# Second MoE: destinations looked up ahead of the gather, and no weight chunk split for an expert that does not exist

## The chip, the cores and the metric

The kernel runs on one core of one Trainium2 chip. The metric is the device time of one execution in microseconds; the time before is 440.69 us, the median of three runs (439.51 to 441.41).

## What is computed

Attention with a local window and global keys (4 x 768 tokens, 8 heads of 64), a soft MoE over its output, and then a second, hard-routed MoE, in which the change lies. All in fp32:

```
def _moe2_ref(x, w_gate, w1, w2):            # x 3072 x 512, 8 experts, F = 1024
    logits = x @ w_gate
    expert_idx = np.argmax(logits, axis=1)
    ...
    gate_w = probs[np.arange(N), expert_idx]
    for e in range(E):
        mask = expert_idx == e
        if not mask.any():
            continue
        xe = x[mask]
        h = np.maximum(xe @ w1[e], 0.0)
        out[mask] = gate_w[mask, None] * (h @ w2[e])
```

## The kernel before

All sizes of the second MoE are found on the chip. Experts that have tokens are numbered by **rank** 0 to used-1. A rank's tokens are cut into **units** of 256 tokens, two **tiles** of 128 each; a rank's last unit may hold only one tile. On these inputs the trace shows 26 scalings (13 units) and 25 stores, and two splits at a rank's end: there are two ranks, the first of 12 units (u = 0 to 11) and the second of one unit (u = 12) with one tile. Every engine runs its own loop over ranks (outer) and units (inner, `u = first + j`), and they meet only in semaphores.

**TensorE** (PE), per unit u: `tile(u, 0)` (8 groups `fc` of 3 matmuls on lines 1626 to 1628, into `Yq[0]`; after `fc == 1` it turns the gathered rows of unit u+1, `turn(u + 1)`, line 1546, which waits for `gathered`), then `hidden(u + 1)` (8 matmuls, line 1557), then `tile(u, 1)`. In `tile(u, 0)` each even `fc` waits for `hid_low` of its quarter of the hidden layer; the last of these waits is before `fc == 6`.

**ScalarE** (ACT): copies the turned rows out (`turned_out`), fetches the folded weights of a coming unit, and makes the four quarters `hh` of the next unit (`relu`, line 1724). At the end of a rank it splits chunks of 128x1024 weights, `raw` to `w2h` (line 1788).

**VectorE** (DVE), per unit: `scaled(u, 0)`, `low(u+1, 0..2)` (line 1913, the low part of the hidden layer, which TensorE waits for as `hid_low`), `scaled(u, 1)`, `low(u+1, 3)`. `scaled` waits until the store before has landed (`stored`), adds one to `row_free`, waits for TensorE's tile, and writes `Ysb` (line 1986). There is one `Ysb`, so a tile's scaling always comes behind the landing of the tile before it. At the end of a rank VectorE forms `w2l` of the chunks that ScalarE split (line 2011).

**GpSimd** (POOL), per unit: `gather(u + 2)`: copy two columns of source rows (`src1`, line 1480), wait for the copy and for `turn(u + 1)`, and issue two indirect DMAs of 128 rows (line 1486). Then for each tile: wait for `row_free`, copy one column of destinations (`dst1`, line 1509), wait for the copy and for `y_scaled`, and issue the indirect store of `Ysb` (line 1513).

How many chunks are split at a rank's end is `chunks_at_end`: four if there is an expert of rank + 2, and otherwise one. ScalarE's one chunk waits for the last quarter of the rank's last tile, VectorE's one for ScalarE's.

Of the kernel before, what the change touches and what calls it, by code (L numbers as in the profile page):

```python
# [15 lines left out]
F32 = mybir.dt.float32  # L16
F32R = mybir.dt.float32r
I32 = mybir.dt.int32
BF16 = mybir.dt.bfloat16
ALU = mybir.AluOpType  # L20
# [3 lines left out]
P = 128  # L24
# [12 lines left out]
TOK = BATCH * SEQ  # L37
# [22 lines left out]
W2CH = 4  # L60
# [1163 lines left out]
def top1_moe(nc, ctx, sb, psum, sem, block, sp_passed, ident, ones, Rsel, wg_sb, mem, STR, CT, counting,  # L1224
# [7 lines left out]
    st = ExitStack()  # L1232
# [4 lines left out]
    dst_i = sb(st, "dst_i", [P, MAXT], I32)  # L1237
# [7 lines left out]
    Ysb = spare[:, 0:D]  # L1245
    Gpart = spare[:, WSIZE - 4 * 512:].rearrange("p (n f) -> p n f", f=512)
    Gall = mem[:, 2:4, :].rearrange("p a (b f) -> p (a b) f", f=F)
    w2h = sb(st, "w2h", [P, 2, WSIZE], F32R)
    w2l = sb(st, "w2l", [P, 2, WSIZE], F32R)
# [2 lines left out]
    Cg = sb(st, "Cg", [P, 2, P])  # L1252
    CgT = sb(st, "CgT", [P, 2 * P], F32R)
    src1 = sb(st, "src1", [P, 2], I32)
    dst1 = sb(st, "dst1", [P, 1], I32)

    GWs = sb(st, "GWs", [P, REP, NE])
    own_rows = sb(st, "own_rows", [P, REP])
# [10 lines left out]
    act = sb(st, "act", [P, NE])  # L1269
# [34 lines left out]
    raw = mem[:, 0, :]  # L1304
# [38 lines left out]
    v2_loaded = [sem("v2_loaded_first"), sem("v2_loaded_second")]  # L1343
# [3 lines left out]
    w2_high = sem("w2_high")  # L1347
    w2_low = sem("w2_low")
    src_copied = sem("src_copied")
    dst_copied = sem("dst_copied")  # L1350
# [6 lines left out]
    y_quarter = sem("y_quarter")  # L1357
    y_first = sem("y_first")
    y_scaled = sem("y_scaled")
    stored = sem("stored")  # L1360
    row_free = sem("row_free")
    g_here = sem("g_here")
    g_kept = sem("g_kept")
    act_passed = sem("act_passed")
    dve_passed = sem("dve_passed")
    pool_step = sem("pool_step")
    tokens_hot = sem("tokens_hot")

    def column(t):

        return t if isinstance(t, int) else t.with_bounds(min_val=0, max_val=MAXT - 2)
# [5 lines left out]
    def rank_at(r):  # L1377

        return r if isinstance(r, int) else r.with_bounds(min_val=0, max_val=NE - 1)
# [5 lines left out]
    def plan(eng, r):  # L1385

        word = eng.value_load(rt[0:1, 1, bass.ds(rank_at(r), 1)], min_val=0, max_val=(1 << 19) - 1)
        return ((word & 15).with_bounds(min_val=1, max_val=TT // 2),
                ((word >> 4) & 31).with_bounds(min_val=0, max_val=MAXU - 3),
                ((word >> 9) & 31).with_bounds(min_val=1, max_val=TT),  # L1390
                (word >> 14).with_bounds(min_val=0, max_val=TT + NE - 2))

    def count(eng):

        return eng.value_load(rt[0:1, 2, 0:1], min_val=1, max_val=NE)

    def all_units(eng):

        return eng.value_load(rt[0:1, 2, 1:2], min_val=1, max_val=MAXU - 2)

    def all_tiles(eng):

        return eng.value_load(rt[0:1, 2, 2:3], min_val=1, max_val=TT + NE - 1)

    def chunks_at_end(rank, used):


        return 1 + (rank + 2 < used) * (W2CH - 1)

    def chunk(ch):  # L1410

        return slice(ch * CW, (ch + 1) * CW) if isinstance(ch, int) else bass.ds(ch * CW, CW)
# [50 lines left out]
    @block.gpsimd  # L1463
    def _(pool):
        pool.sem_inc(y_quarter, 4)
        pool.sem_inc(y_scaled, 2)
        pool.wait_ge(c_stored, 16)
        pool.wait_ge(first_ready, 1)

        def gather(u, turned):  # L1470


            if not isinstance(u, int) or u >= 1:
                pool.wait_ge(gathered, u * 32)
                pool.sem_inc(pool_step, 1)
            if isinstance(u, int):
                index = src_i[:, 2 * u:2 * u + 2] if u else src_0[:]
            else:
                index = src1[:]
                nc.gpsimd.tensor_copy(src1[:], src_i[:, bass.ds(column(u * 2), 2)]).then_inc(src_copied, 1)  # L1480
                pool.wait_ge(src_copied, u - 1)
            if not isinstance(u, int) or u >= 1:
                pool.wait_ge(cg_turned, turned)
            pool.sem_inc(pool_step, 1)
            for i in range(2):
                nc.gpsimd.indirect_dma_start(out=Cg[:, i, :], out_offset=None, in_=c_dram,  # L1486
                                             in_offset=bass.IndirectOffsetOnAxis(ap=index[:, i:i + 1], axis=0)
                                             ).then_inc(gathered, 16)

        gather(0, 0)  # L1490
        pool.wait_ge(v2_half, 16)
        nc.gpsimd.tensor_copy(w2h[:, 0, chunk(0)], w2l[:, 0, chunk(0)].bitcast(F32)).then_inc(w2_first, 1)
        pool.wait_ge(src_ready, 1)
        gather(1, 1)
        pool.wait_ge(rt_ready, 1)
        pool.wait_ge(dst_ready, 1)
        used, total = count(pool), all_tiles(pool)
        with pool.Fori(0, used) as rank:
            units, first, tiles, tile0 = plan(pool, rank)
            with pool.Fori(0, units) as j:  # L1500
                u = first + j
                gather(u + 2, u + 2)

                with pool.Fori(0, 1 + (tiles > j * 2 + 1)) as i:
                    done = tile0 + j * 2 + i

                    pool.wait_ge(row_free, u * 2 + i + 1)
                    pool.sem_inc(pool_step, 1)
                    nc.gpsimd.tensor_copy(dst1[:], dst_i[:, bass.ds(column(u * 2 + i), 1)]).then_inc(dst_copied, 1)
                    pool.wait_ge(dst_copied, done + 1)  # L1510
                    pool.wait_ge(y_scaled, u * 2 + i + 3)
                    pool.sem_inc(pool_step, 1)
                    nc.gpsimd.indirect_dma_start(  # L1513
                        out=out_d, out_offset=bass.IndirectOffsetOnAxis(ap=dst1[:, 0:1], axis=0),
                        in_=Ysb, in_offset=None, bounds_check=TOK - 1, oob_is_err=False
                    ).then_inc(stored, 16)

        pool.wait_ge(stored, total * 16)
        pool.sem_inc(pool_step, 1)
        units = all_units(pool)  # L1520
        pool.wait_ge(gathered, (units + 2) * 32)
        pool.sem_inc(pool_step, 1)
# [166 lines left out]
    def _(act):  # L1689
# [3 lines left out]
        used = count(act)  # L1693
# [86 lines left out]

        def rank_done(rank, last):

            act.wait_ge(v2_loaded[1], (rank + 1) * (rank + 2 < used) * 16 + 16)
            act.sem_inc(act_passed, 1)
            act.wait_ge(y_quarter, last * 4 + 4)
            act.sem_inc(act_passed, 1)
            with act.Fori(0, chunks_at_end(rank, used)) as ch:
                nc.scalar.copy(w2h[:, bass.ds(rank & 1, 1), chunk(ch)].rearrange("p a f -> p (a f)"),
                               raw[:, chunk(ch)]).then_inc(w2_high, 1)

        act.wait_ge(v1_loaded[1], 16)
        for ch in range(W2CH):
# [1 line left out]
        with act.Fori(0, used) as rank:  # L1794
            units, first = plan(act, rank)[0:2]

            with act.If(units > (rank < 1) * 1):
                with act.Fori((rank < 1) * 1, units) as j:
                    u = first + j
# [4 lines left out]
    def _(dve):  # L1804
        v = nc.vector
# [140 lines left out]
        step(v.tensor_reduce(tr_f[:], past[:], AX, ALU.add))  # L1946
        v.tensor_scalar(tr[:], tr_f[:], float(NE - 1), None, ALU.min).then_inc(rt_ready, 1)

        used = count(dve)

        dve.wait_ge(r_exp, 1)
# [21 lines left out]
        def scaled(u, i, done):  # L1973

            if isinstance(done, int):
                if done:
                    dve.wait_ge(stored, done * 16)
            else:
                with dve.If(done > 0):
                    dve.wait_ge(stored, done * 16)  # L1980
                    dve.sem_inc(dve_passed, 1)
            dve.sem_inc(row_free, 1)
            dve.wait_ge(*((y_quarter, u * 4 + 8) if i else (y_first, u + 1)))
            dve.sem_inc(dve_passed, 1)
            at = u * 2 + i
            v.tensor_scalar(Ysb, Yq[i][:], gate_s[:, at:at + 1] if isinstance(u, int) else  # L1986
                            gate_s[:, bass.ds(column(at), 1)], None, ALU.mult).then_inc(y_scaled, 1)
# [7 lines left out]
        with dve.Fori(0, used) as rank:  # L1995
            units, first, _, tile0 = plan(dve, rank)

            with dve.If(units > (rank < 1) * 1):
                with dve.Fori((rank < 1) * 1, units) as j:
                    u = first + j  # L2000
                    scaled(u, 0, tile0 + j * 2)
                    for q in range(3):
                        low(u + 1, q)
                    scaled(u, 1, tile0 + j * 2 + 1)
                    low(u + 1, 3)
            with dve.Fori(0, chunks_at_end(rank, used)) as ch:

                all_done = (rank + 1 < used) + (used < 2)
                dve.wait_ge(w2_high, rank * W2CH + W2CH + 2 + ch + all_done * (W2CH - 1))
                dve.sem_inc(dve_passed, 1)  # L2010
                v.tensor_tensor(w2l[:, bass.ds(rank & 1, 1), chunk(ch)].rearrange("p a f -> p (a f)"), raw[:, chunk(ch)],
                                w2h[:, bass.ds(rank & 1, 1), chunk(ch)].rearrange("p a f -> p (a f)").bitcast(F32),
                                ALU.subtract).then_inc(w2_low, 1)

    st.close()

# [43 lines left out]
```

## Time and profile before

| | us |
|---|---|
| median of three runs | 440.69 |
| lowest, highest | 439.51, 441.41 |
| the profiled execution, its device time | 439.07 |
| its span on the core | 437.40 |
| second MoE's loop over units, from the first store | 287.07 to the end |
| PE busy in the span | 421.4 |
| DVE, ACT, POOL busy | 239.2, 212.2, 210.0 |

The rows below give times in us from the span's start. A timeline row is start, duration, engine, line, operation, output<-input, and in brackets how long the engine had been idle and what released it. A DMA row of POOL is the time in which GpSimd works on the issue, not the transfer. DVEq and POOLq are the sequencers of these engines, which handle semaphores and registers.

### The profile page before, as it was taken

The numbers are of one execution on the slowest core, as the hardware profiler recorded it, in microseconds if no ns is written. First come the engines' busy times: TensorE is split into PE (matmuls) and PEld (weight loads), VectorE is DVE, ScalarE is ACT, GpSimd is POOL, SyncE is SP. The second block draws the span as 40 slices with busy tenths as digits, with TensorE's granted clock in tenths as the row PEclk, the third lists the DMA queues.
The fourth block names the chain that finished last, engine by engine and source line by source line (L and its number), as shares of the span: only waits on it lengthen the run. The fifth ranks groups of instructions, "written<-read, shape, count | busy, mean of one in ns | idle before, by whom it ended". The sixth has DMA issues, their size and how long they took to land.

```text
span 437.4 us, 9412 instructions
## 1 busy us (share of the span) xinstructions
PE 421.4 (96%) x3036; PEld 353.6 (81%) x3037; DVE 239.2 (55%) x791; ACT 212.2 (49%) x418; POOL 210.0 (48%) x216
## 2 busy tenths in 40 slices
PE   8999999999999999998797999999999999999996
PEld 7899999999999997743234977688888888888884
DVE  6667777777767775556100679574333323333344
ACT  3887788788888773422010016373333333332244
POOL 5899999999999910010001020234333344443422
PEclk9999999999999999999999999999999999999999
DMA  7866989898977304999995488511111111112111
GB/s 236 278 220 251 402 345 393 343 364 317 393 262 240 106 21 133 391 391 409 397 386 211 140 294 289 217 55 60 60 53 43 60 60 60 60 36 58 55 54 14
DMA packets 29174, 89.21 MB, mean 204 GB/s; under 512 B 3440, under 2 KB 6000, under 8 KB 29136
## 3 DMA queue, kind: packets, MB, share of 16 engines
q1 hardware_dynamic: 25456, 78.47, 48.4%
q0 software_dynamic: 3360, 9.83, 7.2%
q10 hardware_dynamic: 320, 0.42, 0.4%
q8 instruction: 22, 0.36, 0.3%
q14 instruction: 16, 0.13, 0.1%
HBM read 80.85 MB, written 8.13 MB: 203 GB/s over the span
## 4 chain that ended last, share of the span: by engine, by line
PE 85%; DMA 7%; DVE 3%; issue 2%; ACT 1%; POOL 0%; SPq 0%; ACTq 0%; DVEq 0%; POOLq 0%
PE O L445 17%; PE Yq L1626 11%; PE Yq L1627 10%; PE Yq L1628 10%; PE PT L427 9%; PE S L418 5%; PE S L417 5%; DMA ext<-in_moe_w 5%; PE Gp L1557 3%; DMA w2h<-in_moe_w 2%; PE XTp L893 2%; PE Lp L982 2%; PE Cp L1529 2%; PE O L395 2%; PE Up L902 1%
## 5 line engine op out<-in xcount | busy, mean ns | idle before, releaser
L523 ACT ACTIVATE shared<-shared,nm 128x256 f32<-128x256 f32 (+1 forms) x192 | 83.7, 484 | 30.3 <-DVE nm L636 30.1
L445 PE MATMUL O<-V,PTs 128*128 128x65 f32 x704 | 90.1, 269 | 0.0
L636 DVE CUSTOM_DVE_ANT_0 shared<-S,TA 128x256 f32<-128x256 f32 (+1 forms) x192 | 68.7, 396 | 34.4 <-PE S L418 31.7
L445 PEld LDWEIGHTS O<-V,PTs 128*128 128x128 f32 x704 | 86.5, 191 | 1.1 <-issue 1.0
L1626 PE MATMUL Yq<-w2h,hh 128*128 x208 | 83.0, 399 | 0.4 <-issue 0.4
L1627 PE MATMUL Yq<-w2l,hh 128*128 x208 | 81.2, 390 | 0.0
L1628 PE MATMUL Yq<-w2h,hl 128*128 x208 | 81.2, 390 | 0.0
L380 POOL TENSOR_TENSOR kl<-k_raw,kh 128x816 fp32r<-128x816 f32 x30 | 57.9, 1931 | 5.0 <-ACT kh L538 2.9
L1913 DVE SCALAR_TENSOR_TENSOR hl<-Gp,hh 128x512 fp32r<-128x512 f32 x56 | 38.1, 688 | 39.4 <-ACT hh L1724 39.4
L376 POOL TENSOR_TENSOR qs<-q_raw,qs 64x768 fp32r<-64x768 f32 x30 | 54.7, 1825 | 2.4
L427 PE MATMUL PT<-ident,shared 128*128 128x128 f32 x352 | 54.7, 274 | 0.0
L417 PE MATMUL S<-kh,qs 128*128 128x256 f32 (+1 forms) x180 | 53.0, 317 | 0.0
L1724 ACT ACTIVATE hh<-Gp 128x512 fp32r<-128x512 f32 x56 | 32.9, 600 | 30.4 <-PE Yq L1628 27.4
L1986 DVE TENSOR_SCALAR mem<-Yq,gate_s 128x512 f32<-128x512 f32 x26 | 19.5, 751 | 49.7 <-PE Yq L1628 47.0
L1626 PEld LDWEIGHTS Yq<-w2h,hh 128*128 128x128 f32 x208 | 39.1, 188 | 9.2 <-issue 1.5
L418 PE MATMUL S<-kl,qs 128*128 128x256 f32 (+1 forms) x180 | 46.2, 280 | 0.0
L1628 PEld LDWEIGHTS Yq<-w2h,hl 128*128 128x128 f32 x208 | 39.0, 188 | 8.3
L1627 PEld LDWEIGHTS Yq<-w2l,hh 128*128 128x128 f32 x208 | 39.2, 188 | 7.4 <-issue 0.2
L1486 POOL DMA_INDIRECT Cg<-c_rows,src x28 | 27.6, 986 | 35.2 <-DVE src L1892 19.6
L1513 POOL DMA_INDIRECT out<-mem,dst x25 | 25.5, 1019 | 37.4 <-DVE mem L1986 34.4
L1736 ACT CAST Gst<-mem 128x512 fp32r x28 | 16.0, 617 | 54.7 <-PE Gp L1557 53.3
L427 PEld LDWEIGHTS PT<-ident,shared 128*128 128x128 f32 x352 | 42.1, 156 | 0.3 <-ACT shared L523 0.3
(248 smaller groups left out, 571.7 us busy)
## 6 DMA issues: line engine op xcount, KB each, us to landing
mem<-in_moe_w SPq DMA_DIRECT2D x9, 2048.0 KB, 11.6
ext<-in_moe_w SPq DMA_DIRECT2D x6, 2048.0 KB, 19.8
V<-in_v SPq DMA_DIRECT2D x16, 715.0 KB, 6.8
k_raw<-in_k SPq DMA_DIRECT2D x13, 816.0 KB, 7.0
q_raw<-in_q SPq DMA_DIRECT2D x13, 768.0 KB, 4.6
xmem<-in_moe_w SPq DMA_DIRECT2D x2, 2048.0 KB, 11.1
w2h<-in_moe_w SPq DMA_DIRECT2D x1, 2048.0 KB, 10.2
w2l<-in_moe_w SPq DMA_DIRECT2D x1, 2048.0 KB, 15.5
```

The costliest lines, as they stand in the source:

```text
L376: nc.gpsimd.tensor_tensor(qs[HD:P, buf, :, cq], q_raw[HD:P, buf, :, cq], qs[HD:P, buf, :, cq].bitcast(F32), ALU.subtract).then_inc(q_split, 1)
L380: nc.gpsimd.tensor_tensor(kl[:, buf, :, ck], k_raw[:, buf, :, ck], kh[:, buf, :, ck].bitcast(F32), ALU.subtract).then_inc(k_split, 1)
L417: pe.matmul(S[par][h][:, 0:w], q, kh[:, buf, h, at:at + w], start=True, stop=False)
L418: mm = pe.matmul(S[par][h][:, 0:w], q, kl[:, buf, h, at:at + w], start=False, stop=True)
L427: mm = pe.transpose(PT[par][:, (h * kbs + kb) * P:(h * kbs + kb + 1) * P], Pb[:, par, h, kb * P:(kb + 1) * P], ident[:])
L445: mm = pe.matmul(O[grp % 2][:, at:at + VC], PTs[:, par, (h * kbs + kb) * P:(h * kbs + kb + 1) * P], V[:, buf, h, vb, :], start=(n == 0), s ...
L523: nc.scalar.activation(Pb[:, par, h, 0:width(g)], Pb[:, par, h, 0:width(g)], ACT.Exp, bias=nm[:, par, h:h + 1], scale=-1.0).then_inc(exp_d ...
L636: v.tensor_tensor_reduce(Pb[:, par, h, 0:w], S[par][h][:, 0:w], tab, -SCALE, HUGE, ALU.add, ALU.min, nm[:, par, h:h + 1]).then_inc(biased, 1)
L1626: pe.matmul(Yq[i][:], h, high[:, cols], start=(fc == 0), stop=False)
L1627: pe.matmul(Yq[i][:], h, low[:, cols], start=False, stop=False)
L1628: mm = pe.matmul(Yq[i][:], rest, high[:, cols], start=False, stop=(fc == FC - 1))
L1913: v.scalar_tensor_tensor(hl[:, q, :], Gp[:, q, :], 0.0, hh[:, q, :].bitcast(F32), ALU.max, ALU.subtract).then_inc(hid_low, 1)
```

## The change

GpSimd's loop over a unit's tiles is written out. At the start of a unit it waits for `row_free` of the unit's first tile (the landing of the last store of the unit before), copies two columns of destinations at once, then runs `gather(u + 2)`, then the stores; the second store has no copy and no wait for `row_free` any more. So that the first unit doesn't wait for its own tile, VectorE adds the first `row_free` ahead of the loop. `chunks_at_end` goes away: ScalarE and VectorE split four chunks if there is an expert of rank + 2, and otherwise none.

```diff
-    dst1 = sb(st, "dst1", [P, 1], I32)
+    dst1 = sb(st, "dst1", [P, 2], I32)
...
+        def store(i):
+            nc.gpsimd.indirect_dma_start(
+                out=out_d, out_offset=bass.IndirectOffsetOnAxis(ap=dst1[:, i:i + 1], axis=0),
+                in_=Ysb, in_offset=None, bounds_check=TOK - 1, oob_is_err=False).then_inc(stored, 16)
...
             with pool.Fori(0, units) as j:
                 u = first + j
+                pool.wait_ge(row_free, u * 2 + 1)
+                pool.sem_inc(pool_step, 1)
+                nc.gpsimd.tensor_copy(dst1[:], dst_i[:, bass.ds(column(u * 2), 2)]).then_inc(dst_copied, 1)
                 gather(u + 2, u + 2)
-                with pool.Fori(0, 1 + (tiles > j * 2 + 1)) as i:
-                    done = tile0 + j * 2 + i
-                    pool.wait_ge(row_free, u * 2 + i + 1)
...
-                    pool.wait_ge(dst_copied, done + 1)
-                    pool.wait_ge(y_scaled, u * 2 + i + 3)
...
+                pool.wait_ge(dst_copied, u + 1)
+                pool.wait_ge(y_scaled, u * 2 + 3)
+                pool.sem_inc(pool_step, 1)
+                store(0)
+                with pool.If(tiles > j * 2 + 1):
+                    pool.wait_ge(y_scaled, u * 2 + 4)
                     pool.sem_inc(pool_step, 1)
+                    store(1)
...
         def rank_done(rank, last):
-            act.wait_ge(v2_loaded[1], (rank + 1) * (rank + 2 < used) * 16 + 16)
...
-            with act.Fori(0, chunks_at_end(rank, used)) as ch:
+            with act.If(rank + 2 < used):
...
+                for ch in range(W2CH):
...
+        dve.sem_inc(row_free, 1)
         used = count(dve)
...
-            dve.sem_inc(row_free, 1)
+            if not isinstance(done, int) or done:
+                dve.sem_inc(row_free, 1)
...
-            with dve.Fori(0, chunks_at_end(rank, used)) as ch:
+            with dve.If(rank + 2 < used):
+                for ch in range(W2CH):
```

GpSimd, the body of the loop over units, before. `src` and `dst` are `src1` and `dst1`, the first two DMAs the gather, `out<-mem` the store:

```order
L1480 COPY src<-src_i 128x2
L1481 REGISTER_ALU
L1486 DMA Cg<-c_rows,src 128x128 [waits src_copied,cg_turned]
L1486 DMA Cg<-c_rows,src 128x128
L1504 UNCONDITIONAL_BRANCH
L1504 ISA
L1509 ISA [waits row_free]
L1509 COPY dst<-dst_i 128x1
L1510 ISA
L1511 REGISTER_ALU [waits dst_copied]
L1513 DMA out<-mem,dst 3072x512 [waits y_scaled]
```

The same place after:

```order
L1506 ISA [waits row_free]
L1506 COPY dst<-dst_i 128x2
L1469 ISA
L1475 ISA [waits gathered]
L1475 COPY src<-src_i 128x2
L1476 REGISTER_ALU
L1481 DMA Cg<-c_rows,src 128x128 [waits src_copied,cg_turned]
L1481 DMA Cg<-c_rows,src 128x128
L1509 REGISTER_ALU [waits dst_copied]
L1487 DMA out<-mem,dst 3072x512 [waits y_scaled]
```

The wait for `row_free` and the copy of destinations moved from behind the two gather DMAs to ahead of them, and nothing but a register operation is left between the gather and the first store.

ScalarE, the end of the loop over ranks, before (`w2h<-mem` is the split of a chunk of `raw`):

```order
L1785 REGISTER_ALU [waits v2_loaded_second]
L1785 REGISTER_ALU
L1785 ISA
L1787 UNCONDITIONAL_BRANCH [waits y_quarter]
L1787 ISA
L1788 REGISTER_ALU
L1788 ISA
L1788 COPY w2h<-mem 128x1024
```

The same place after:

```order
L1784 REGISTER_ALU
L1784 COMPARE_AND_BRANCH
L1785 ISA
L1787 REGISTER_ALU [waits v2_loaded_second]
L1787 REGISTER_ALU
L1787 ISA
L1790 REGISTER_ALU [waits y_quarter]
L1790 ISA
L1790 COPY w2h<-mem 128x1024
```

A branch now stands ahead of the waits and the copy, and jumps over all of it for the last two ranks; VectorE's end of a rank is changed in the same way.

## Rows read from the trace of the kernel before

**Rows 1.** The page: PE's share of the span, and the chain that ended last.
```profile
PE 421.4 (96%) x3036; PEld 353.6 (81%) x3037; DVE 239.2 (55%) x791; ACT 212.2 (49%) x418; POOL 210.0 (48%) x216
...
PE 85%; DMA 7%; DVE 3%; issue 2%; ACT 1%; POOL 0%; SPq 0%; ACTq 0%; DVEq 0%; POOLq 0%
```

**Rows 2.** The chain that ended last, its final pieces: start, us, what.
```profile
432.87 0.24 PE Yq L1628
...
434.31 1.05 ACT w2h L1788
...
435.87 1.22 DVE w2l L2011
```

**Rows 3.** Timeline, VectorE at the end: last scaling, last `low`, the chunk's low half.
```profile
433.35 0.75 DVE L1986 TENSOR_SCALAR mem<-Yq,gate_s 128x512 f32<-128x512 f32 x1 [0.19 <-PE Yq L1628]
434.02 0.68 DVE L1913 SCALAR_TENSOR_TENSOR hl<-Gp,hh 128x512 fp32r<-128x512 f32 x1
435.87 1.22 DVE L2011 TENSOR_TENSOR w2l<-mem,w2h  x1 [1.17 <-ACT w2h L1788]
```

**Rows 4.** The chain: the hidden matmuls of two units ten units apart.
```profile
305.55 0.95 PE Gp L1557 x8
...
426.68 0.95 PE Gp L1557 x8
```

**Rows 5.** Timeline, GpSimd in units 0 to 2: stores, lookups and one whole gather.
```profile
291.80 1.08 POOL L1513 DMA_INDIRECT out<-mem,dst  x1 [1.45 <-DVE mem L1986]
...
297.61 1.02 POOL L1513 DMA_INDIRECT out<-mem,dst  x1 [0.99 <-POOL dst L1509]
300.77 0.18 POOL L1509 COPY dst<-dst_i 128x1 int32 x1 [2.14 <-DVEq L1982]
302.59 1.00 POOL L1513 DMA_INDIRECT out<-mem,dst  x1 [1.63 <-DVE mem L1986]
303.60 0.20 POOL L1480 COPY src<-src_i 128x2 int32 x1
304.65 0.98 POOL L1486 DMA_INDIRECT Cg<-c_rows,src  x1 [0.85 <-POOL src L1480]
305.94 0.97 POOL L1486 DMA_INDIRECT Cg<-c_rows,src  x1 [0.30 <-issue]
306.91 0.20 POOL L1509 COPY dst<-dst_i 128x1 int32 x1
```

**Rows 6.** Timeline, VectorE: the scaling of unit 1's second tile, and of unit 2's.
```profile
300.92 0.75 DVE L1986 TENSOR_SCALAR mem<-Yq,gate_s 128x512 f32<-128x512 f32 x1 [1.01 <-DMA out<-mem,dst]
...
312.22 0.75 DVE L1986 TENSOR_SCALAR mem<-Yq,gate_s 128x512 f32<-128x512 f32 x1 [0.19 <-PE Yq L1628]
```

**Rows 7.** VectorE's sequencer passing the wait for `stored`, in three windows: last numbers are starts.
```profile
L1981 DVEq EVENT_SEMAPHORE  x1: 21/21/21, 294.6 to 294.6; - x1
...
L1981 DVEq EVENT_SEMAPHORE  x1: 21/21/21, 300.4 to 300.4; - x1
...
L1981 DVEq EVENT_SEMAPHORE  x1: 21/21/21, 305.4 to 305.4; - x1
```

**Rows 8.** All gather DMAs: landing after their start, and GpSimd's register work behind a lookup, ns.
```profile
DMA to landing us min/median/max: 2.5/2.6/3.8
...
L1510 POOLq FUSED_REGOPS  x25: 163/165/167, 285.0 to 426.6; - x25
```

**Rows 9.** Timeline, TensorE's weight loads in unit 2: the gathered rows, and `fc == 6`.
```profile
300.83 0.37 PEld L1546 LDWEIGHTS Cp<-ident,Cg 128*128 128x128 f32 x2
...
303.80 0.19 PEld L1626 LDWEIGHTS Yq<-w2h,hh 128*128 128x128 f32 x1
```

**Rows 10.** Timeline, the turn from rank 0 to rank 1: the other splits, and what follows.
```profile
422.21 1.05 ACT L1788 CAST w2h<-mem  x1 [0.53 <-issue]
...
423.78 1.23 DVE L2011 TENSOR_TENSOR w2l<-mem,w2h  x1 [1.19 <-ACT w2h L1788]
...
424.72 0.33 POOL L1480 COPY src<-src_i 128x2 int32 x1 [0.81 <-issue]
...
426.94 0.75 DVE L1986 TENSOR_SCALAR mem<-Yq,gate_s 128x512 f32<-128x512 f32 x1 [1.94 <-PE Yq L1628]
```

**Rows 11.** Timeline, GpSimd: the last store of all.
```profile
429.37 1.03 POOL L1513 DMA_INDIRECT out<-mem,dst  x1 [0.99 <-POOL dst L1509]
```

More of the change, by code:

```diff
@@ L1403, in all_tiles @@
         return eng.value_load(rt[0:1, 2, 2:3], min_val=1, max_val=TT + NE - 1)
-    def chunks_at_end(rank, used):
-        return 1 + (rank + 2 < used) * (W2CH - 1)
     def chunk(ch):
@@ L1498, in _ @@
         with pool.Fori(0, used) as rank:
-            units, first, tiles, tile0 = plan(pool, rank)
+            units, first, tiles, _ = plan(pool, rank)
             with pool.Fori(0, units) as j:
                 u = first + j
+                pool.wait_ge(row_free, u * 2 + 1)
+                pool.sem_inc(pool_step, 1)
+                nc.gpsimd.tensor_copy(dst1[:], dst_i[:, bass.ds(column(u * 2), 2)]).then_inc(dst_copied, 1)
                 gather(u + 2, u + 2)
-                with pool.Fori(0, 1 + (tiles > j * 2 + 1)) as i:
-                    done = tile0 + j * 2 + i
-                    pool.wait_ge(row_free, u * 2 + i + 1)
-                    pool.sem_inc(pool_step, 1)
-                    nc.gpsimd.tensor_copy(dst1[:], dst_i[:, bass.ds(column(u * 2 + i), 1)]).then_inc(dst_copied, 1)
-                    pool.wait_ge(dst_copied, done + 1)
-                    pool.wait_ge(y_scaled, u * 2 + i + 3)
[L1512 to L1516, printed above, removed]
+                pool.wait_ge(dst_copied, u + 1)
[4 more added lines that the diff above has]
+                    pool.wait_ge(y_scaled, u * 2 + 4)
+                    pool.sem_inc(pool_step, 1)
+                    store(1)
         pool.wait_ge(stored, total * 16)
@@ L1781, in rank_done @@
         def rank_done(rank, last):
-            act.wait_ge(v2_loaded[1], (rank + 1) * (rank + 2 < used) * 16 + 16)
-            act.sem_inc(act_passed, 1)
-            act.wait_ge(y_quarter, last * 4 + 4)
-            act.sem_inc(act_passed, 1)
-            with act.Fori(0, chunks_at_end(rank, used)) as ch:
-                nc.scalar.copy(w2h[:, bass.ds(rank & 1, 1), chunk(ch)].rearrange("p a f -> p (a f)"),
-                               raw[:, chunk(ch)]).then_inc(w2_high, 1)
+            with act.If(rank + 2 < used):
+                act.wait_ge(v2_loaded[1], rank * 16 + 32)
+                act.sem_inc(act_passed, 1)
+                act.wait_ge(y_quarter, last * 4 + 4)
+                act.sem_inc(act_passed, 1)
+                for ch in range(W2CH):
+                    nc.scalar.copy(w2h[:, bass.ds(rank & 1, 1), chunk(ch)].rearrange("p a f -> p (a f)"),
+                                   raw[:, chunk(ch)]).then_inc(w2_high, 1)
         act.wait_ge(v1_loaded[1], 16)
@@ L2005, in _ @@
                     low(u + 1, 3)
-            with dve.Fori(0, chunks_at_end(rank, used)) as ch:
[L2008 to L2013, printed above, removed]
+            with dve.If(rank + 2 < used):
+                for ch in range(W2CH):
+                    dve.wait_ge(w2_high, rank * W2CH + (2 * W2CH + ch + 1))
+                    dve.sem_inc(dve_passed, 1)
+                    v.tensor_tensor(w2l[:, bass.ds(rank & 1, 1), chunk(ch)].rearrange("p a f -> p (a f)"),
+                                    raw[:, chunk(ch)],
+                                    w2h[:, bass.ds(rank & 1, 1), chunk(ch)].rearrange("p a f -> p (a f)").bitcast(F32),
+                                    ALU.subtract).then_inc(w2_low, 1)
     st.close()
```

## The prediction

> **What bounds the kernel now.** I read the page first, then the end of the chain, then the timelines of GpSimd and VectorE inside a unit. TensorE is busy for 421.4 of 437.4 us and has 85% of the chain [rows 1]. In the second MoE its hidden matmuls stand 121.13 us apart over ten units [rows 4], so a unit takes 12.11 us, and the chain there is PE piece after PE piece. GpSimd, VectorE and ScalarE only have to keep up.
>
> Two places are different. First the end. TensorE's last matmul begins at 432.87, but the chain goes on through a chunk split by ScalarE (434.31, 1.05 us) and its low half on VectorE (435.87, 1.22 us) [rows 2]. VectorE had finished its last real work, the `low`, at 434.02 + 0.68 = 434.70; the low half ends at 437.09, and the span 0.31 later [rows 3]. No expert of rank + 2 exists, so nobody reads that chunk: 2.39 us of the span are waste.
>
> Second, what GpSimd and VectorE do to each other. There is one `Ysb`, so store and scaling alternate. A store that starts at 291.80, 297.61 or 302.59 [rows 5] lets VectorE's sequencer past its wait at 294.6, 300.4 and 305.4 [rows 7]: 2.8 us each time. Now the gather runs inside that time, since GpSimd starts it right behind a unit's second store (302.59 + 1.00, then the source copy at 303.60) [rows 5]. By unit 2 VectorE waits for TensorE alone when it scales a second tile (312.22, 0.19 us) [rows 6]: there is slack in that ring.
>
> **Part 1: the split that goes.** At the very end both halves go, 2.39 us. What is late next is the `low` at 434.70, if it stays where it is, and 0.31 us of closing work as now: a span of 435.01. VectorE gets a branch in place of a loop of one turn; I take it at nothing, for it runs in the sequencer while the 0.68 us `low` is still busy. If that cover failed it would be some tenths.
>
> The same pair goes at the turn of ranks, at 422.21 and 423.78. VectorE was idle for 1.94 us behind it, waiting for a tile of TensorE (426.94) [rows 10]. That is worth nothing. Where an expert of rank + 2 exists the work is the same; with two ranks it never runs.
>
> **Part 2: the lookup that moves.** Two things come off GpSimd between stores: the copy ahead of the second store, which stood in the wait for TensorE's tile and costs nothing today, and the copy between gather and first store (0.20 and 0.99 us) [rows 5]. One thing is added: the wait for `row_free` ahead of the gather. Behind it are queued on GpSimd the destination copy, the source copy, both gather DMAs and the first store; TensorE waits for the gather, VectorE for the store's landing, and through VectorE's in-order queue TensorE's `hid_low` waits too. What lay side by side, the landing of the second store and the gather, now lies in a row. The ring of one unit, each term from a start to the next start:
>
> - destination copy to source copy: 0.30. The copy takes 0.20; I add 0.10, since register work of the kind that takes 0.165 [rows 8] partly runs beside it. Bounds 0.20 and 0.45.
> - source copy to the end of the second gather DMA: 306.91 - 303.60 = 3.31 [rows 5].
> - to the first store: 0.30, as between the two gather DMAs. The other bound is 0.99, the gap from a copy to a store [rows 5]. I take 0.30, since both waits of this store are met while the gathers are still being issued, so the sequencer can hand it over early; a copy directly behind a gather starts with no gap at all (306.91).
> - first store to the scaling of the second tile: 300.92 - 297.61 = 3.31 [rows 5, 6], the landing and the restart of VectorE. TensorE's tile is done by then.
> - that scaling to the second store: 302.59 - 300.92 = 1.67.
> - second store to the next destination copy: 3.16, as from 297.61 to 300.77 [rows 5].
>
> The sum is 12.05 us, against TensorE's 12.11. So the ring just keeps pace, with 0.06 us in hand per unit, where it had several us.
>
> **How late it starts.** Unit 0 is as before: its lookup comes free at once, its second store at 291.80 is bound by VectorE. VectorE passes its wait at 294.6 [rows 7] and the destination copy follows at 291.80 + 3.16 = 294.96; source copy 295.26, gather issued by 298.57, store 298.87, scaling of unit 1's second tile 302.18. If TensorE alone set that scaling it would stand one unit ahead of 312.22, at 300.11. So the ring starts 2.07 us late. Does TensorE notice? The second gather DMA starts at 295.26 + 0.20 + 0.85 + 0.98 + 0.30 = 297.59 and lands 2.6 later [rows 5, 8], at 300.19; TensorE loads these rows at 300.83 [rows 9]. And `low(2, 3)` ends 1.35 us behind the start of the scaling (433.35 to 434.70 in [rows 3]), at 303.53, while the group that needs it loads at 303.80 [rows 9]. It fits, by 0.27 us. TensorE keeps its 12.11.
>
> **At the end** the lateness is 2.07 - 11 x 0.06 = 1.38 (302.18 + 11 x 12.05 = 434.73 against 433.35). The last `low` ends at 436.08, the span at 436.39. GpSimd itself is done earlier: its last store starts at 434.73 - 3.31 = 431.42 (now 429.37 [rows 11]) and lands 2.8 later, with one register load behind it, of the kind that left 0.81 us idle at the turn of ranks [rows 10]. The turn itself costs the ring nothing: 0.81 is less than the 2.8 of a landing.
>
> So the change gives 2.39 and takes back 1.38: **-1.0 us**. Against the profiled execution that is 439.07 to 438.06, its span from 437.40 to 436.39, with the 1.67 between the two unchanged. The median of the runs lies 1.62 above the profiled one; there I expect 439.7.
>
> **A rule of the skill against these rows.** The rows say 2.8 us from a store's start until its landing is seen, and 2.6 for a gather. The Trainium skill, "DMA: Bandwidth & Descriptors", section "Anatomy of one DMA — SWDGE (gpsimd) path", gives about 2.0 us plus the bytes at 436 GB/s and lays most of the fixed part to the receipt of the write. By that page, as an estimate, a store of 256 KB would take 2.6 us and a gather of 64 KB 2.15, the ring would be 11.65 us and the whole lateness would be gone by the end, the first rival below; the trace is 0.2 longer per store, and I follow it. The page also speaks against the change itself, since a receipt that nothing shortens is put in front of the gather.
>
> **Rivals.**
>
> *The ring catches up.* If it is 11.92 us or shorter, the 2.07 us are gone by unit 12 and the last `low` stands at 434.70: span 435.01, -2.4 us, 438.3 in the median. It needs 0.13 less in a sum of six terms; for it speaks that the copies could overlap fully (0.1), against it that all three landings read 2.8. Chance 0.16, in which the page's figures count a little.
>
> *The ring is a little longer than TensorE's unit*, 12.11 to 12.35, because the store's transfer now follows the gather's on the same queue at 1.3 us where it followed at 2.2 or more. At 12.25 the last scaling is at 302.18 + 134.75 = 436.93 and the span ends at 438.6: +1.2 us, 441.9. The end's gain is eaten and TensorE, which has 0.27 us of slack, begins to wait for `hid_low` in the middle units. Between no change and +2.2. Chance 0.22.
>
> *The store is not handed over early.* If the 0.99 us stays between gather and store, the ring is 12.74, and it starts 0.69 later: 302.87 + 140.14 = 443.0 for the last scaling, span 444.7, +7.3 us, 448.0. This ends on the slower side; it decides from a ring of about 12.3 upward, and its mark is TensorE idle at `fc == 6` in every unit. Against it speaks that the copy behind the gathers has no gap. Chance 0.09.
>
> *Nothing moves*: the end is held by some other closing work within a few tenths of 437.4. VectorE's row is the last there is, and ScalarE and GpSimd end before. Chance 0.03.
>
> **How the numbers follow.** The forecast, a ring of 11.92 to 12.11, has 0.50: 438.4 to 440.7 in the median. About 0.5% (2.2 us) is what a measurement of this kernel tells from no change. Of the first rival about three quarters lie beyond it, which gives faster 0.12; slower is the third rival and a rim of the second, 0.12; the rest is same, 0.76. The range leaves out the third rival and the rims: 437.9 to 442.5.
>
> **What would show it.** No row of ScalarE or VectorE behind the last `low`. Each unit's destination copy ahead of its source copy, 3.2 us behind a store's start; first store 0.3 us behind the second gather DMA. VectorE's second scaling released by the store's landing, not by TensorE, in most units, and its distance to TensorE's tile shrinking by 0.06 a unit. TensorE's units still 12.11 apart: if they are longer, the slack argument is wrong; if the last scaling stands at 433.4, the ring is shorter than I added up.

## The result

The changed kernel takes 442.69 us in the median of 12 runs (441.37 to 445.3) against 439.84 us (438.57 to 441.41, 12 runs) of the kernel before: a ratio of 1.0066, 95% interval 1.0047 to 1.0085. It is slower, by 2.9 us in the medians and by 2.3 us between the two profiled executions (439.07 and 441.37). Forecast were 1.0 us less, to 439.7, and a range that ended at 442.5. The profiled execution of the changed kernel is the fastest of its 12, so the traces show the small end of the loss.

The page of the changed kernel, to hold against [rows 1]: the engines' line, the chain by engine, and its first lines of code.

```profile
span 439.7 us, 9240 instructions
...
PE 422.6 (96%) x3036; PEld 353.4 (80%) x3037; DVE 237.1 (54%) x789; ACT 210.2 (48%) x416; POOL 207.0 (47%) x204
...
PE 38%; DMA 26%; issue 13%; POOL 12%; DVE 6%; POOLq 2%; DVEq 1%; ACT 1%; SPq 0%; ACTq 0%
DMA out<-mem,dst 15%; PE O L445 11%; PE PT L427 6%; DMA ext<-in_moe_w 5%; POOL Cg L1481 4%; POOL kl L380 4%; PE S L418 3%; POOL qs L376 3%; PE S L417 3%; DMA w2h<-in_moe_w 2%; DVE mem L1991 2%; PE XTp L893 2%; PE Lp L982 2%; DMA k_raw<-in_k 2%; PE Cp L1529 2%
```

TensorE had 85% of the chain and has 38%; the landings of stores, GpSimd and the gaps of issue have taken its place (of GpSimd's 12%, 7 are `kl` and `qs` of the attention and not this loop). TensorE's pace in the loop is unchanged: its hidden matmuls of the same two units as in [rows 4] start at 304.98 and 426.12, 121.14 us apart, and both stand 0.4 us earlier than before. The 1.2 us that it is busy longer in all (421.4 and 422.6 us) lie ahead of the loop: between 200 and 240 us it was busy for 35.7 us at a granted clock of 0.96, before for 33.7 at 1.00.

One unit of the changed kernel in GpSimd's timeline (start, us, engine, line, operation, what released it); [rows 5] is the same stretch before:

```profile
303.45 1.00 POOL L1487 DMA_INDIRECT out<-mem,dst  x1 [3.95 <-DVE mem L1991]
306.58 0.18 POOL L1506 COPY dst<-dst_i 128x2 int32 x1 [2.13 <-DVEq L1987]
306.87 0.18 POOL L1475 COPY src<-src_i 128x2 int32 x1
307.90 1.00 POOL L1481 DMA_INDIRECT Cg<-c_rows,src  x1 [0.85 <-POOL src L1475]
309.20 0.97 POOL L1481 DMA_INDIRECT Cg<-c_rows,src  x1 [0.30 <-issue]
310.48 1.02 POOL L1487 DMA_INDIRECT out<-mem,dst  x1 [0.30 <-issue]
315.45 1.00 POOL L1487 DMA_INDIRECT out<-mem,dst  x1 [3.95 <-DVE mem L1991]
```

The ring is there as the prediction drew it, and it takes 315.45 - 303.45 = 12.00 us (12.05 was added up). The destination copy waits for the landing, the gather for the copy, the first store stands 0.30 us behind the gather. VectorE waits for stores and not for TensorE; from its waits, over the second MoE:

```profile
DVE mem L1991 <- DMA out<-mem,dst: 63.4, 24, 3.7
...
POOL dst L1506 <- DVEq L1987: 25.6, 12, 2.2
```

And the end of both, VectorE's last two operations of the changed kernel (against [rows 3]):

```profile
434.45 0.75 DVE L1991 TENSOR_SCALAR mem<-Yq,gate_s 128x512 f32<-128x512 f32 x1 [1.69 <-DMA out<-mem,dst]
435.12 0.68 DVE L1915 SCALAR_TENSOR_TENSOR hl<-Gp,hh 128x512 fp32r<-128x512 f32 x1
```

The last scaling begins at 434.45 (434.73 forecast), the last `low` ends at 435.80, and yet the span ends at 439.7, 3.9 us later. What fills this time is in no timeline of busy work. It is in the rows of the sequencers on the line that closes the program, L129. There each engine's sequencer runs one DRAIN, and in both traces the closing semaphores of all engines come behind the last of these. The rows give how long each one drained (ns), and when it began. First GpSimd and VectorE before:

```profile
L129 POOLq DRAIN  x1: 4655/4655/4655, 432.5 to 432.5; - x1
...
L129 DVEq DRAIN  x1: 791/791/791, 436.4 to 436.4; - x1
```

then after the change:

```profile
L129 POOLq DRAIN  x1: 4655/4655/4655, 434.8 to 434.8; - x1
L129 DVEq DRAIN  x1: 676/676/676, 435.2 to 435.2; - x1
```

In both traces GpSimd drains for 4.655 us once it has nothing left. Before, that ended at 437.15, beside VectorE's chunk at 437.09 and VectorE's own drain at 437.2: these starts are given to 0.1 us, so the two ends were level, and the chain showed one of them. After, it ends at 439.45, the span 0.25 later, as before, while every other engine is through by 435.9. So GpSimd's last wait, which is for the last store, counts one for one, and VectorE's `low` has over 3 us to spare.

The ledger of the profiled pair: the last store starts at 431.19 where it started at 429.37 [rows 11], +1.82, though the whole changed run is 0.50 ahead by then (first store at 286.57, before 287.07), so the loop itself has lost 2.32. The last store is seen landed at 433.9, before at 431.7: 2.7 and not 2.3 us after its start, +0.4 to 0.5. Together 2.3 on the span.

### The profile page after: what moved, and what is told of

Same layout as the page of the kernel before. It is cut to its first block, busy times and chain, and to the rows that moved or that the text cites. A ratio compares the mean times of both kernels' runs of the same rounds, so it can differ in the third digit from the quotient of the medians.

```text
span 439.7 us, 9240 instructions
## 1 busy us (share of the span) xinstructions
PE 422.6 (96%) x3036; PEld 353.4 (80%) x3037; DVE 237.1 (54%) x789; ACT 210.2 (48%) x416; POOL 207.0 (47%) x204
## 4 chain that ended last, share of the span: by engine, by line
PE 38%; DMA 26%; issue 13%; POOL 12%; DVE 6%; POOLq 2%; DVEq 1%; ACT 1%; SPq 0%; ACTq 0%
DMA out<-mem,dst 15%; PE O L445 11%; PE PT L427 6%; DMA ext<-in_moe_w 5%; POOL Cg L1481 4%; POOL kl L380 4%; PE S L418 3%; POOL qs L376 3%; PE S L417 3%; DMA w2h<-in_moe_w 2%; DVE mem L1991 2%; PE XTp L893 2%; PE Lp L982 2%; DMA k_raw<-in_k 2%; PE Cp L1529 2%
```

## Experiments

**What holds the end.** Theory A: GpSimd's drain behind its last wait. Theory B, the prediction's: VectorE's chunk. First the one half of the change that drops the splits, on ScalarE and VectorE, with GpSimd as before:

```diff
-            with act.Fori(0, chunks_at_end(rank, used)) as ch:
+            with act.If(rank + 2 < used):
...
-            with dve.Fori(0, chunks_at_end(rank, used)) as ch:
+            with dve.If(rank + 2 < used):
...
```

> The kernel before with the one part of the change that drops the chunk splits at a rank's end; GpSimd as before. Theory A (the end is GpSimd's: it waits for the last store, then drains for 4.655 us in both traces, ending at 437.15 before and 439.45 after; VectorE's chunk ended at 437.09 beside it): no change, 0.0 us, at most -0.1. Theory B (the prediction's: VectorE's chunk sets the end): -2.4 us.

Measured: 0.9993 of before (0.998 to 1.0005). Its profile, the drains of GpSimd and VectorE:

```profile
L129 POOLq DRAIN  x1: 4655/4655/4655, 433.1 to 433.1; - x1
...
L129 DVEq DRAIN  x1: 316/316/316, 435.2 to 435.2; - x1
```

VectorE is done at 435.5, GpSimd at 437.8, the span is 437.9. The 2.39 us of splits are gone from VectorE and nothing is gained. Theory B is out.

The other half alone, GpSimd's loop with the splits kept:

```diff
+                pool.wait_ge(row_free, u * 2 + 1)
+                pool.sem_inc(pool_step, 1)
+                nc.gpsimd.tensor_copy(dst1[:], dst_i[:, bass.ds(column(u * 2), 2)]).then_inc(dst_copied, 1)
                 gather(u + 2, u + 2)
...
```

> The kernel before with GpSimd's loop of the change alone; the chunk at a rank's end is split as before. Theory A: the last store starts at about 431.2 in place of 429.4 and lands some tenths slower, so the whole loss of the change stands here alone: +2.3 us or a little more. Theory B: VectorE's last chunk follows the last low by nothing, so the end moves by the 1.0 us that the last scaling is late, or not at all: 0 to +1.0 us.

Measured: 1.0063 (1.0044 to 1.0083), 443.26 us in the median; the change as a whole is at 1.0066. All of the loss is in this half.

Now the lookup back behind the gather, everything else of the change kept:

```diff
+                gather(u + 2, u + 2)
                 pool.wait_ge(row_free, u * 2 + 1)
                 pool.sem_inc(pool_step, 1)
                 nc.gpsimd.tensor_copy(dst1[:], dst_i[:, bass.ds(column(u * 2), 2)]).then_inc(dst_copied, 1)
-                gather(u + 2, u + 2)
```

> The changed kernel with one thing moved back: the wait for row_free and the lookup of both destinations stand behind the gather again, the second store still has no lookup of its own. Theory A: the ring's lateness is gone, the last store starts at 429.4 as before, and the time is that of before: 0.0 us (+-0.3) against before, 2.3 less than the change. Theory B (no split at the end counts): -2.4 us against before. If the time were as slow as the change, the place of the lookup would not be the cause.

Measured: 0.9992 (0.997 to 1.0014). Its last store:

```profile
429.24 1.03 POOL L1487 DMA_INDIRECT out<-mem,dst  x1 [0.99 <-POOL dst L1507]
```

Looking up two destinations at once costs and brings nothing that shows; it is the place ahead of the gather, with the wait that it needs, that costs the whole 2.9 us.

**Is the drain movable?** Without the splits, and with the last wait given to SyncE:

```diff
+        sp.wait_ge(rt_ready, 1)
+        total = all_tiles(sp)
+        sp.wait_ge(stored, total * 16)
+        sp.sem_inc(sp_passed, 1)
...
-        pool.wait_ge(stored, total * 16)
-        pool.sem_inc(pool_step, 1)
...
```

> The kernel before without the splits at a rank's end, and with the wait for all stores moved from GpSimd to SyncE, which is idle since 266 us. Theory A: GpSimd's drain starts when its last DMA issue and the last gather have passed (430.4, not 432.5) and ends near 435.1; the last low of VectorE ends at 434.7: -2.1 us. If the drain were the wait for outstanding stores, and not a fixed 4.655 us, or if it began no earlier, nothing moves. Theory B: -2.4 us as without the splits alone.

Measured: 0.9972 (0.9955 to 0.9988), -1.2 us by the ratio, less than the 2.1 forecast, but clear of before where the splits alone were not. The intervals of these two runs touch, so it is the trace that carries the reading:

```profile
L129 POOLq DRAIN  x1: 4655/4655/4655, 430.9 to 430.9; - x1
L129 SPq DRAIN  x1: 13/13/13, 431.6 to 431.6; - x1
```

The drain begins at 430.9, before the stores are seen landed (SyncE passes at 431.6), and takes 4.655 us again. Its length doesn't change with the landing's place, and it goes on 4 us behind the landing, so it is not a wait for the stores. It ends at 435.55, the profiled span is 435.8 against 437.4, 1.6 less; GpSimd began its drain 0.5 later than I had put it.

A control in the other direction, work added on GpSimd between its last wait and the drain:

```diff
         pool.wait_ge(stored, total * 16)
         pool.sem_inc(pool_step, 1)
+        late = nc.gpsimd.tensor_copy(work[:, 0:1024], work[:, 1024:2048].bitcast(F32))
```

> The kernel before with one GpSimd copy of 128x1024 numbers (1.04 us in the trace for the same shape) between its last wait and its drain. Theory A (GpSimd's drain of 4.655 us holds the end): +1.0 us. Theory B (VectorE's chunk holds it): 0.

Measured: 1.0006 (0.9993 to 1.0019), which does not tell 0 from +0.5 us, and it is not the +1.0 of theory A as I wrote it. The profile says why:

```profile
432.49 1.05 POOL L1520 CAST work<-work 128x1024 fp32r<-128x1024 f32 x1 [1.41 <-DMA out<-mem,dst]
...
L129 POOLq DRAIN  x1: 4988/4988/4988, 433.2 to 433.2; - x1
```

The copy ran beside the register load that stands there anyway, so it put off the end of GpSimd's work by 0.3 us only. The drain began at 433.2 with the copy still running, and ended at 438.19, 4.65 us behind the copy's end (433.54). So with work still running the drain lasts 4.65 us from that work's end; with none running (seven of the other traces) it lasts 4.655 us from its own start. As a timing the run is inconclusive.

**Why more is lost than the ring's lateness.** The landings of stores in the changed kernel, from the chain (start, us, what): one of the many, then the two first stores of units 10 and 11, and the last.

```profile
310.48 2.78 DMA out<-mem,dst
...
406.45 3.06 DMA out<-mem,dst
...
418.73 3.28 DMA out<-mem,dst
...
431.19 2.74 DMA out<-mem,dst
```

The two in the middle land 0.3 and 0.5 us late, and the last takes 2.7 us where it took 2.3 before; in the ring a late landing is lateness. The profile of the run with GpSimd's half alone shows worse, its first and second store of unit 11 at 4.65 and 3.46 us. That execution was the slowest of its seven (446.47, the median 443.26), and its second store stands 6.8 us behind the first and not right behind a gather; why that one took 3.46 us no run shows. The two stores:

```profile
421.44 4.65 DMA out<-mem,dst
...
428.28 3.46 DMA out<-mem,dst
```

There TensorE did wait for `hid_low`:

```profile
428.20 0.49 PE L1631 MATMUL Yq<-w2h,hh 128*128 x1 [0.36 <-DVE hl L1918]
```

The kernel before already shows where the late first stores come from. The landing of the two gathers that GpSimd issued in a middle unit, and of the two that it issued in unit 11, for unit 13, each with GpSimd's rows of them:

```profile
L1486 POOL DMA_INDIRECT Cg<-c_rows,src x2: 970/980/989, 340.2 to 341.5; - x2
...
DMA to landing us min/median/max: 2.6/2.6/2.6
```

```profile
L1486 POOL DMA_INDIRECT Cg<-c_rows,src x2: 970/981/992, 412.9 to 414.2; - x2
...
DMA to landing us min/median/max: 3.6/3.7/3.8
```

From unit 10 on a gather fetches units 12, 13 and 14, which hold few tokens or none (the store of unit 12's one tile moves 0.02 MB where another moves 0.24 to 0.26); the source of every padded row is `max(0 - 1, 0)`, row 0. Theory C: rows that all read one address are slow, and the store queued right behind them waits. To tell it from the rival, that the late landings belong to the end of a rank, the padded rows read 128 different rows instead:

```diff
-        v.tensor_scalar(src_i[:], Sp[:, 0:MAXT], -1.0, 0.0, ALU.add, ALU.max).then_inc(src_ready, 1)
+        step(v.tensor_scalar(sf[:, 2, :], Sp[:, 0:MAXT], 0.5, tok[:, 0:1], ALU.is_lt, ALU.mult))
+        v.scalar_tensor_tensor(src_i[:], Sp[:, 0:MAXT], -1.0, sf[:, 2, :], ALU.add, ALU.add).then_inc(src_ready, 1)
```

> The changed kernel, with the padded rows of a tile gathered from 128 different rows of the combine weights in place of row 0 for all (two small VectorE operations in place of one; what is gathered there is never stored). Theory C (the landings of 3.1 to 4.7 us of the stores of units 10 and 11 come from standing behind gathers whose padded rows all read one row of HBM; these gathers land in 3.7 us and not 2.7 in the kernel before too): stores behind them land in 2.8 us again, the last store starts 0.8 us earlier or more, so -0.8 us against the changed kernel and no runs above 443 us: +0.4 to +0.5% against before in place of +0.65%. Rival D (the slow landings have to do with the end of the rank or with other traffic): landings and time as in the changed kernel, +0.65%.

It costs VectorE one small operation more, ahead of the loop. Measured: 1.0036 (1.0022 to 1.005), and no run above 443.12 where the change had 445.3. The same landings:

```profile
406.86 2.79 DMA out<-mem,dst
...
418.87 2.77 DMA out<-mem,dst
...
430.82 2.27 DMA out<-mem,dst
```

Theory C holds: all landings are ordinary, the last one 2.3 us as in the kernel before, and 1.3 us of the 2.9 are back by the ratios. Their intervals (1.0022 to 1.005 and 1.0047 to 1.0085) still overlap a little, but the traces agree: the three landings are 0.27, 0.51 and 0.47 us shorter, 1.25 in all. The profile gives no landing of the gathers themselves for this run; their packets show it. The packets of each of the two gathers for unit 13 are spread over about 1.0 us in the changed kernel and over about 0.35 us here. What is left, some 1.6 us, is the ring's lateness and the gather in front of the last store.

**The gather in front of the last store.** It is the gather of unit 14, and nobody uses its rows. Left out of the changed kernel:

```diff
-                gather(u + 2, u + 2)
+                with pool.If(u + 1 < real):
+                    gather(u + 2, u + 2)
```

> The changed kernel without the gather of the unit after the last hidden layer (u + 2 = 14), whose rows nobody uses. Theory A: the last store follows its scaling (start near 429.3 in place of 431.2, lands in 2.3), GpSimd drains 2.3 us earlier: the time of the kernel before, 0 to +0.2%. If the lateness of the ring alone were what costs, whatever stands between, it would stay at +2 us.

Measured: 1.0024 (1.0007 to 1.0041), just above the 0 to +0.2% that theory A gave, and slower than before. The last store has no gather ahead of it any more. But the ring got longer by the branch:

```profile
398.12 1.02 POOL L1487 DMA_INDIRECT out<-mem,dst  x1 [0.30 <-issue]
...
406.64 0.18 POOL L1475 COPY src<-src_i 128x2 int32 x1 [0.24 <-issue]
...
410.24 1.02 POOL L1487 DMA_INDIRECT out<-mem,dst  x1 [0.30 <-issue]
...
425.58 0.20 PEld L1546 LDWEIGHTS Cp<-ident,Cg 128*128 128x128 f32 x2 [0.89 <-DMA Cg<-c_rows,src]
...
433.43 0.98 POOL L1487 DMA_INDIRECT out<-mem,dst  x1 [1.74 <-DVE mem L1991]
```

410.24 - 398.12 = 12.12 us, no less than TensorE's 12.11, so nothing of the lateness was worked off, and the slow padded gather of unit 13 (its two DMAs landed in 3.6 and 4.2 us, the second from 421.39) then made TensorE itself wait, 0.89 us at 425.58. The last store starts at 433.43 (the run was 1.9 us behind that of before when the loop began). This run shows how near the edge the ring stands: 0.12 us of register work took all that was in hand. The profiled execution is one of the slower of its twelve (442.35, the median 441.35), so how often TensorE waited in the others is not known, and no run tells the ring's lateness and the gather in front of the last store apart.

**A version that beats both**: the lookup behind the gather, no splits, no gather for unit 14, and SyncE waits for the stores (the edits of the runs with the lookup behind, with SyncE's wait and without the last gather together).

> Lookup of both destinations behind the gather, no split at a rank's end, no gather for the unit after the last, and SyncE in place of GpSimd waits for the stores. Theory A: last store starts at 428.6, GpSimd's drain starts near 430.3 and ends near 435.0, level with VectorE's last low (434.7): span 435.1, -2.3 us against before, 1.0 to 1.3 us faster than with SyncE's wait alone (which gave -1.0). Theory B (the drain is a wait for the stores to land, so that it can't end before them and moves with them): no better than that version.

Measured: 0.9952 (0.9934 to 0.9971), 438.15 us in the median, -2.1 us against before, about as forecast.

```profile
428.89 0.98 POOL L1491 DMA_INDIRECT out<-mem,dst  x1 [2.41 <-DVE mem L1993]
...
434.33 0.68 DVE L1917 SCALAR_TENSOR_TENSOR hl<-Gp,hh 128x512 fp32r<-128x512 f32 x1
...
L129 POOLq DRAIN  x1: 4852/4852/4852, 429.5 to 429.5; - x1
```

GpSimd is through at 434.35, VectorE's `low` at 435.01, the span is 435.3. Only here is the end that the prediction reasoned about the real one. Dropping the splits can be worth something once GpSimd is through ahead of 437.1, where VectorE's chunk ended before. That is so here and in the run with SyncE's wait (435.55); neither was run with the splits kept, so what they are worth there is not shown.

## Why the prediction was wrong

**What bounds the end: wrong, and this is the step that failed.** "2.39 us of the span are waste" took the last row of the chain for the only end. The chain follows one of the engines back; GpSimd's drain of 4.655 us ended level with VectorE's chunk (437.15 and 437.09) and is in no row of busy work. So the term of -2.39 us was worth nothing: the splits alone gave 0.9993.

**"GpSimd itself is done earlier": wrong for the same reason.** I had its last store nearly right (431.42 put, 431.19 found in a run that was 0.50 ahead, so 0.27 later) and its register load, and stopped there. With the drain the same sum gives the loss: 2.05 us later than before on a path that sets the end, in place of 1.0 us gained.

**The ring: right.** 12.00 us found, 12.05 added up; first store 0.30 behind the gather. TensorE was not stopped in the profiled execution, and the slack at the start was enough. The last scaling, 434.45 against 434.73, stands closer than it should, and that is luck. TensorE was 0.4 us ahead in this run, so the scaling was 1.5 us late against TensorE where 1.38 was forecast; a ring that is 0.05 shorter would have taken off 0.6 more over 11 units, and the two late landings put 0.8 back. (2.07 - 11 x 0.06 is 1.41; the 1.38 comes from the times beside it.)

**The landings: a term left out.** [rows 8] has a maximum of 3.8 us beside the median of 2.6, and I used the median for all. The slow gathers are the padded ones, all at the end, right ahead of stores that count. Spreading their rows gave back 1.3 of the 2.9 us.

**The rivals.** The first needed a ring of 11.92 us and the third a store that isn't handed over early; neither occurred. The second had the right sign, but by another mechanism. None had GpSimd's end as the bound: "the end is held by some other closing work" stood at 0.03 and claimed that ScalarE and GpSimd end before. By the fit in the Trainium skill, "DMA: Bandwidth & Descriptors", section "Anatomy of one DMA — SWDGE (gpsimd) path", a store of 256 KB takes 2.6 us, as an estimate; the traces have 2.75 to 2.8 for nearly all, and 2.3 for the last one, which moves only 0.02 MB, when no slow gather is ahead of it. The same section of the Trainium skill lays most of the fixed cost to the receipt of the write. How a landing divides no run here shows; the whole of it, put ahead of the gather, is paid in the ring.

## What to carry to other kernels

Look for every engine's closing work before you price the end: list the sequencers' rows on the program's last line, and take the latest end, not the last busy row of the chain. A lookup moved ahead of a transfer takes its wait along; if that wait is for a landing, two transfers that lay side by side are now in a row, so compare the new ring with the unit of the engine that sets the pace, and expect anything late in it to reach the end. Padding that reads one address is not free.

## What the runs showed of the hardware

- GpSimd's drain at the end of the program took 4.655 us in seven of the ten traces, in one of them begun before the stores had landed (430.9). Of the other three, one had 4.49 us (the run without the last gather), and in two GpSimd still had work at the drain's start: it ran 4.5 and 4.65 us from that work's end (4.852 and 4.988 in all). TensorE's took 3.7 us, VectorE's took 0.3 to 0.8 us, SyncE's 0.013.
- An indirect gather of 128 rows of 512 bytes landed 2.6 us after its start in the middle units and 3.5 to 3.9 us when nearly all rows were the same one (in the traces before and after); a store that GpSimd started 0.3 us behind such a gather landed in 3.06 to 4.65 us in place of 2.8, and in 2.79 and 2.77 when the rows were spread.
- The last store, of 0.02 MB, landed in 2.2 to 2.3 us where stores of 0.24 to 0.26 MB took 2.7 to 2.8.
- GpSimd started a third indirect DMA 0.30 us behind the second although two semaphore waits stood between them, when both had been met early.
